# Loading the first gated layer's weights one by one during the last attention pair but one

## What is computed

```python
q_rot, k_rot = rotate(q), rotate(k)                      # rotary embedding
scores = q_rot @ k_rot.T / sqrt(64)
attn = exp(scores - max); attn /= (sum(attn) + 1e-9)
x = (attn @ v)  -> [2304 tokens, 512]
x = (sigmoid(x @ w_gate) * (x @ w_val)) @ w_out          # first gated layer, d_ff 1536
h = x @ w_in2; solu = h * softmax(h)                     # second layer, d_ff 1024
y = (layernorm(solu) * g_ln) @ w_out2
```

## Time and profile before

| | |
|---|---|
| median of 3 runs | 959.44 us (957.44 to 960.39) |
| the profiled execution | 958.99 us |
| its span | 957.2 us |
| PE busy | 943.4 us, 99% |
| DVE busy | 475.0 us, 50% |
| ACT busy | 371.3 us, 39% |
| POOL busy | 338.8 us, 35% |
| PE's share of the chain that ended last | 90% |
| mean granted TensorE clock | 0.997 |
| DMA queue that SP and the loads use (q1) | 35632 packets, 47.53 MB, 18.1% of 16 engines |

### The profile page before, as it was taken

How to read it: one execution, slowest core, us unless ns; L and a number is a source line. 1 busy time by engine, 2 the same in 40 slices (tenths; PEclk the granted TensorE clock), 3 DMA queues, 4 the chain that set the end, 5 groups by cost and what they waited for, 6 DMA issues and landing times.

```text
span 957.2 us, 15347 instructions
## 1 busy us (share of the span) xinstructions
PE 943.4 (99%) x5346; PEld 787.2 (82%) x5346; DVE 475.0 (50%) x859; ACT 371.3 (39%) x801; POOL 338.8 (35%) x246
## 2 busy tenths in 40 slices
PE   8999999999989999999999999999999999999998
PEld 6787888888777889888888888888888888888886
DVE  6787888788753243323324233243434554444441
ACT  6887888888853111111111111111111343333332
POOL 5455647465405805104203302401756432222200
PEclk9999999999999999999999999999999999999999
DMA  3435343343422100200100100100120011000112
GB/s 95 128 86 136 90 128 101 104 121 85 116 93 81 40 27 1 67 0 1 66 1 1 67 1 0 44 0 0 45 86 1 1 23 22 22 22 22 22 22 45
DMA packets 35810, 48.14 MB, mean 50 GB/s; under 512 B 6592, under 2 KB 22208, under 8 KB 35776
## 3 DMA queue, kind: packets, MB, share of 16 engines
q1 hardware_dynamic: 35632, 47.53, 18.1%
q10 hardware_dynamic: 144, 0.15, 0.1%
HBM read 33.02 MB, written 5.31 MB: 40 GB/s over the span
## 4 chain that ended last, share of the span: by engine, by line
PE 90%; DMA 3%; issue 2%; DVE 1%; ACT 1%; POOL 1%; SPq 1%; DVEq 0%; ACTq 0%; POOLq 0%
PE ps L1145 31%; PE ps L1189 15%; PE ps L1252 10%; PE ps L1227 9%; PE ps L1127 8%; PE ps L1085 7%; PE ps L1109 6%; PE ps L1237 2%; DMA rrep<-inverses 1%; PE ps L1053 1%; DMA inverses<-rinv_t 1%; PE ps L1024 1%; DMA raw_q<-in_q 1%; DVE nmax L889 0%; SPq L506 0%
## 5 line engine op out<-in xcount | busy, mean ns | idle before, releaser
L1145 PE MATMUL ps<-x_hi,w_hi 128*128 128x512 f32 (+1 forms) x480 | 177.0, 369 | 0.0
L1145 PE MATMUL ps<-x_lo,w_hi 128*128 128x512 f32 (+1 forms) x480 | 176.7, 368 | 0.0
L1145 PE MATMUL ps<-x_hi,w_lo 128*128 128x512 f32 (+1 forms) x480 | 176.6, 368 | 0.0
L953 DVE TENSOR_TENSOR hid<-ps,sig 128x512 f32<-128x512 f32 (+1 forms) x60 | 38.3, 638 | 243.1 <-PE ps L1145 214.6
L767 ACT ACTIVATE sig<-ps 128x512 f32<-128x512 f32 (+1 forms) x60 | 33.3, 555 | 299.6 <-PE ps L1145 299.6
L889 DVE TENSOR_REDUCE nmax<-ps 128x1 f32<-128x576 f32 x144 | 107.1, 752 | 37.7 <-PE ps L1085 37.6
L1085 PE MATMUL ps<-kT,qT 128*128 128x288 f32 x640 | 120.7, 314 | 3.0 <-ACT prob L735 2.2
L637 POOL TENSOR_SCALAR w_hi<-raw_w 128x1024 fp32r<-128x1024 f32 x15 | 41.3, 2775 | 215.5 <-PE ps L1189 215.5
L1085 PEld LDWEIGHTS ps<-kT,qT 128*128 128x128 f32 x640 | 89.5, 189 | 17.8 <-ACT prob L735 10.3
L1145 PEld LDWEIGHTS ps<-x_hi,w_hi 128*128 128x128 f32 x480 | 90.5, 189 | 15.4 <-issue 0.5
L1145 PEld LDWEIGHTS ps<-x_hi,w_lo 128*128 128x128 f32 x480 | 90.5, 189 | 15.0
(11 more groups left out here) (117 smaller groups left out, 1611.2 us busy)
## 6 DMA issues: line engine op xcount, KB each, us to landing
kT<-kT SPq DMA_DIRECT2D x30, 304.0 KB, 4.6
raw_k<-in_k SPq DMA_DIRECT2D x16, 288.0 KB, 3.8
raw_q<-in_q SPq DMA_DIRECT2D x16, 288.0 KB, 4.9
rrep<-inverses SPq DMA_DIRECT2D x16, 288.0 KB, 3.8
out_y<-y_sb SPq DMA_DIRECT2D x36, 128.0 KB, 2.3
v_sb<-in_v SPq DMA_DIRECT2D x64, 64.0 KB, 2.3
raw_w<-in_moe_w_gate SPq DMA_DIRECT2D x6, 512.0 KB, 3.7
raw_w<-in_moe_w_val SPq DMA_DIRECT2D x6, 512.0 KB, 4.6
```

The costliest lines, as they stand in the source:

```text
L1145: last = nc.tensor.matmul(in_parts(gv_ps[f][n][:, 0:size(c)], c), w, x, start=m == 0, stop=m == len(todo) - 1)
```

## The change

The three loads of group 0 leave step 15 and go to step 14, each at another place of SP's order: w_gate behind the reciprocals' spreading (RR), behind a wait that POOL has rotated all 16 pairs' keys and queries; w_val behind the exchange (T); w_out behind V's loads (LV), behind the wait for the last turned tiles, which stood in step 15 before. The helper `weights(g)` keeps its three DMAs, now through `weight(g, n)`. Nothing else is changed: DVE still waits for all three before it makes the first high part.

```diff
--- before.py
+++ after.py
@@ -489,12 +489,20 @@
             parts = [w_gate.rearrange("(k p) f -> p k f", p=P), w_val.rearrange("(k p) f -> p k f", p=P)]
             rows = w_out.rearrange("(f p) n -> p f n", p=P)
 
+            def weight(g, n):
+                if n < 2:
+                    src, dst = parts[n][:, :, bass.ds(g * (GF * P), GF * P)], raw_w[:, n, :].rearrange("p (k f) -> p k f", k=KT)
+                else:
+                    src, dst = rows[:, bass.ds(g * GF, GF), :], raw_w[:, n, :].rearrange("p (f n) -> p f n", f=GF)
+                sp.dma_start(dst, src).then_inc(w_in_g, 16)
+
             def weights(g):
-                for n in range(2):
-                    sp.dma_start(raw_w[:, n, :].rearrange("p (k f) -> p k f", k=KT),
-                                 parts[n][:, :, bass.ds(g * (GF * P), GF * P)]).then_inc(w_in_g, 16)
-                sp.dma_start(raw_w[:, 2, :].rearrange("p (f n) -> p f n", f=GF),
-                             rows[:, bass.ds(g * GF, GF), :]).then_inc(w_in_g, 16)
+                for n in range(3):
+                    weight(g, n)
+
+            def last_turned():
+                for bank, before in newest(PIECES, PAIRS - 1):
+                    sp.wait_ge(tr_full[bank], before + 1)
 
             def write_inverses(p, step):
 
@@ -514,10 +522,6 @@
                 sp.dma_start(rrep[:], src).then_inc(rrep_in, 16)
 
             def step_in(name, p, step):
-                if step == PAIRS - 1 and name == "RW":
-                    for bank, before in newest(PIECES, PAIRS - 1):
-                        sp.wait_ge(tr_full[bank], before + 1)
-                    weights(0)
                 if name == "LK":
                     load(p, k, raw_k, k_in, k_prod)
                 elif name == "LQ":
@@ -530,6 +534,15 @@
                     write_inverses(p, step)
                 elif name == "RR":
                     spread_inverses(p)
+                if step == PAIRS - 2 and name == "RR":
+                    sp.wait_ge(k_rot, PAIRS)
+                    sp.wait_ge(q_rot, PAIRS)
+                    weight(0, 0)
+                if step == PAIRS - 2 and name == "T":
+                    weight(0, 1)
+                if step == PAIRS - 2 and name == "LV":
+                    last_turned()
+                    weight(0, 2)
 
             load(0, k, raw_k, k_in, k_prod)
             sp.dma_start(sin_k[:].rearrange("p t d -> p (t d)"), rope[1]).then_inc(sin_in, 16)
```

## The result

The changed kernel takes 954.50 us (median of 13 runs, 953.24 to 955.47), the kernel before, in as many runs beside it, 957.44 us (956.00 to 960.41). The ratio is 0.9966, 95% interval 0.9958 to 0.9975: 2.9 us by the medians, 3.3 by the ratio. The forecast was 955.1, and a gain of 4.3. The two profiled executions differ by more than the medians: their spans are 957.2 and 952.6 us. One execution on record, of the kernel before beside behind2 and again2, took 1049 us at a mean granted clock of 0.851 and is left out of every figure.

What follows compares the result with a forecast made beforehand. PE was taken as the bound nearly everywhere, idle only in step 15's seam. Gains of 2.7 (stall) and 1.7 (clock) less 0.1 made 4.3 us off 958.99, so 954.7, or 955.1 for the median; range 953.6 to 958.4.

Steps and rivals of the forecast that it cites:

- The stall in the seam: Step 15: with earlier reciprocals, PV1 of pair 14 starts at 276.6 instead of 279.33 us; gain 2.7, bounds 2.0 to 3.2.
- DVE's stop: Seam: DVE's 3.03 us wait for all three weights goes; PE's 1.23 us ahead of S6 not counted again.
- PE itself next in line: Seam: PE needs at most 5.84 us from PV0 to PV1, so PV1 starts at most at 276.59.
- the 0.31: Seam: gap in us from the last weight's landing to the spreading's issue, added to w_out's expected landing to give 272.18.
- The clock: Behind PE's gaps in the seam: clock stays up, PV1's 16 matmuls take 2.37 for 4.07 us; gain 1.7, bounds 0 to 1.70.
- The time: Whole kernel: 4.3 us off the profiled 958.99 gives 954.7; forecast for the median 955.1.
- w_gate ahead of the exchange: Step 14: the exchange lands later but still before its score tile; cost nothing, cover 1.4 to 2.8 us.
- The spreading of pair 13's reciprocals behind w_gate: Step 14: w_gate slows the spreading by 0.66 us, of which 0.1 shows; bounds 0 and 0.7.
- The low clock: First rival, seam: w_out still holds the reciprocals and clock falls, 957.5 us; clock alone, 956.8; together chance 0.17.
- no stall moved to step 16: Second rival: something else held the multiply, or the stall reappears in step 16; gain 0 to 1 us, chance 0.09.
- The late exchange: Third rival, start of step 15: exchange lands after its score tile's 265.75; up to 963 us, chance 0.05.

Runs made afterwards that it cites:

- behind2: Changed kernel with all three weight loads behind the exchange and ahead of V's loads, run beside the unedited changed kernel; 954.66 us, ratio to the kernel before 0.9963.
- again2: The changed kernel unedited, run on one chip beside the version with all three loads behind the exchange; 954.43 us, ratio to the kernel before 0.9960.
- nostop: Kernel before, with DVE's first two weight conversions behind the maxima of S5 and S6 instead of S3 and S4; 957.85 us, ratio 0.9999.
- two: Changed kernel with only w_gate loaded early; w_val and w_out stay ahead of pair 14's reciprocals; 953.74 us, ratio to the kernel before 0.9961.
- same: The kernel before, unedited, executed and profiled once more; 957.23 us, ratio 1.0003.
- fill: Kernel before, with seven extra matmuls of zeros in PE's gap ahead of PV1 of pair 14; 956.50 us, ratio 0.9986.
- again: The changed kernel unedited, run once more; 954.68 us against 958.91 for the kernel before on the same chip, ratio 0.9961.
- extra1b: Second profile of the changed kernel with w_gate's 512 KB loaded once more ahead of the exchange, on another chip; one run, 954.92 us.
- behind: Changed kernel with all three weight loads behind the exchange and ahead of V's loads, first run; 953.62 us, ratio to the kernel before 0.9949.
- extra3: Changed kernel with w_gate's 512 KB loaded three more times into unused memory ahead of the exchange; 960.63 us, ratio to the kernel before 1.0023.

## Why the prediction was right, and where it missed

*The stall in the seam* (2.7 us, bounds 2.0 to 3.2). Right: 2.90 us between the two first profiles (8.58 to 5.68), 2.38 against the other profile of the kernel before (8.06). The working was right in its parts too: spreading 3.34 us behind the copy where 3.70 was taken (268.48 to 272.18), DVE's stop inside the same stretch (nostop), and PE itself next in line, which arrives at 5.68 where at most 5.84 was said. Of the 2.02 us that three loads cost between the first write's issue and the spreading's (5.38 for 3.36), the forecast left 0.31 for one load; it cost nothing in the first profile (3.31), where w_out took 0.53 us to issue and landed after 3.7, and not 1.47 and 4.9, which the forecast had taken from w_gate. In again2 it took 1.37 and 4.5, and the spreading came at 3.77, as forecast within 0.1. The second load costs 0.75 (two). What stands behind the 0.31, that the writes land right behind the last weight, is true of the first profile only: in same and fill they had landed 0.7 us before it.

*The clock* (1.7 us). This is the term that was mis-sized. The mechanism was right, and in an execution like the profiled one so was the size: PV1 took 4.07 for 2.37 us, and from the start of PV1 to the first gated product it is 9.20 us for 11.00, so 1.80 in all. The clock now holds in all 30 executions of the changed kernel. But the prediction took one profile's low clock for a property of every execution. It is there in 64 of 95. Counted at that frequency, 0.67, the 1.7 us are 1.1, and the forecast would have been 2.7 + 1.1 − 0.1 = 3.7; with the stall at its mean over the two profiles, 2.6, it is 3.6. Measured are 2.9, 3.6 and 4.2 us by the medians beside the kernel before (first runs, again2, again), and 3.5 between the means of all 95 and all 30 executions (958.1 and 954.6), which were not all on the same chips.

One part of this stays open. By the seams the gain should be 17.24 − 14.88 = 2.36 us in an execution without a low clock and 4.70 in one like the first profile. The changed kernel's mean (954.6) lies 1.9 below the executions without a low clock (956.4) and 4.3 below those with one (958.9); that the latter equals the forecast's sum is chance. The 0.4 to 0.5 us that are missing in either case were not looked into. Chips differ, and so do single executions in what lies around the seam: PV0 of pair 14 starts anywhere from 269.1 to 272.3 us in the profiles without extra loads, and the stretch behind the first gated product takes 666.3 to 666.4 us in five profiles (the first of the changed kernel, fill, nostop, two, extra1b) and 666.8 to 666.9 in the other nine.

*The time.* That 955.1 came so near to 954.50 is in part luck. The forecast started from 959.44, the median of three executions, which is 2.0 us above the median of the thirteen that include them (957.44), and took off 4.3, which is 1.4 more than the medians show. The two errors partly cancel and leave 0.6. They may have one source, since executions with a low clock are the slower ones; the clocks of those three are not on record.

*w_gate ahead of the exchange* (nothing, with a cover of 1.4 to 2.8 us). The cost was right: step 14 is 16.60 us as before. The exchange came 1.4, 1.7 and 2.8 us later in the three profiles, which is just the 1.4 to 2.8 that the working took for the delay. What was mis-sized is the price of a load beyond the first: taken at 1.4 us by its bytes, one more delays the later transfer by 2.0 and 3.7 us against the first profile (8.4 and 10.1 for 6.4), and PE waits 0.3 and 1.8 us. The bytes alone don't tell its landing: with none, one, two and four loads ahead of it, it took 3.8 to 4.1, 5.2 to 6.7, 7.7 to 8.7 and 9.9 us. Whether loads behind it slow it is open: with three right behind it and none ahead (behind) it took 4.0, but with one ahead it took 5.2 where none followed (two) and 5.3 to 6.7 where one or two did.

*The spreading of pair 13's reciprocals behind w_gate* (0.1 us). Nothing: the multiply comes 3.70 us behind the spreading's issue for 3.56, so 0.14 later where 0.66 was taken, and PV1 of pair 13 starts 5.83 us behind PV0, for 5.84.

*The rivals.* The low clock was not seen again in the changed kernel, nor in two, which still has an idle 0.56 us ahead of PV1, and no stall moved to step 16. The late exchange did not happen, though it was near: the estimate of its cover in again2 is 0.4 us. extra3 shows it, 6 us above the changed kernel.

## What to carry to other kernels

A transfer that nobody waits for yet still costs, through what is issued behind it in the same queue: here 36 KB of reciprocals behind 1.5 MB of weights. Move such loads behind the urgent transfers, as in the runs behind and behind2, rather than merely earlier; in time the two could not be told apart here, but the first keeps the exchange's cover, since each load ahead of a deadline uses up cover that one profile overstates. And before a low clock, or anything else that one profiled execution shows behind a short gap, is put into a sum, look at how many executions have it.

## What the runs showed of the hardware

The clock falls behind the same gap in some executions and not in others: PE idle for 1.23 + 1.60 us within some 4 us was followed by 0.50, idle for 1.63 + 0.69 us was not, and over the runs the mean clock was low in two of three. Seven matmuls of zeros in the second gap were enough to hold the clock in 12 of 12. In nostop, whose profile has one gap of 2.53 us with 0.50 behind it, the clock was low in 10 of 12. In extra3 it was low in 9 of 12, but the profiled execution has a gap of 3.29 us and stays at 1.00 behind it. So the length of the gap alone does not tell what an execution will do.

The issue of w_gate's 512 KB took SP 1.47 us in the first profile of the kernel before and 0.53 in the same place in same, fill and nostop, and the spreading was issued 6.48 us behind the copy with the long one and 5.88 to 5.96 with the short one. In the changed kernel w_out took 0.53 (twice) or 1.37 there, with 3.33 to 3.34 or 3.77. What makes the issue long was not tried.
